# Attention and two mixture layers on one core: the experts' scores from operands split into a rounded and a low part

## The chip, the cores and the metric

The kernel runs on one core of one Trainium2 chip. The metric is the device time of one execution in microseconds (us), the median over several executions. Names of the engines: TensorE (PE, with its weight loads as PEld), VectorE (DVE), ScalarE (ACT), GpSimd (POOL), SyncE (SP).

## The reference

Three layers follow each other over a batch of 4, 576 positions and 512 features: a windowed attention of 8 heads, a gated feed-forward layer (products with `w_r`, `w_k`, `w_v`), and a layer of four attention experts with heads of 64. The last one is where the change is made:

```python
logits = x @ w_gate
topk = np.argpartition(-logits, K, axis=-1)[..., :K]      # K = 2
...
for e in range(E):                                        # E = 4
    q = x @ wq[e]
    k = x @ wk[e]
    v = x @ wv[e]
    scores = scale * (q @ k.transpose(0, 2, 1))
    scores = np.where(causal, -1000000000.0, scores)
    scores = scores - scores.max(-1, keepdims=True)
    a = np.exp(scores)
    a /= a.sum(-1, keepdims=True) + 1e-09
    ye = a @ v @ wo[e]
    ...
        out += mask[..., None] * w[:, :, kk:kk + 1] * ye
```

`wq` and `wk` are drawn large, so the scores are large numbers whose differences count.

## The kernel before, in words

Each engine has one program written out by hand, and semaphores order them. The batch loop runs four times. In one batch the dense stage (`pe_dense`) makes the gated layer for two halves of 288 positions, with the next batch's windowed attention put between its units; then comes the experts' stage (`pe_experts`).

All dense products and projections are made in three passes. `pe_passes` (L505 to L509) multiplies rounded by rounded (L507), rounded weights by low part (L508) and low weights by rounded (L509); both parts have the type float32r, and a low part is what rounding took away. The scores of the experts are made otherwise: keys and queries are kept as whole fp32 in `c_kq` and multiplied by a plain fp32 matmul, for which the trace shows two TensorE records each.

The experts' stage, in the order of TensorE:

- Projections, in the order of `PROJECTIONS`: kq 0 to 3, v 0 to 4, kq 4 to 7, twelve passes each. "kq n" is half n % 2 of the positions, of keys (n // 2 even) or queries (odd), for the pair of experts n // 4. They go through two PSUM banks `MM`; a bank may be filled again when `mm_out` of it has counted up, and ACT's `act_projection` (L851 to L863) empties it and counts: L863 writes `c_kq`, L859 writes `c_v`.
- Scores come in ten tiles k = 0 to 9 (`TILES`), five for each pair: 128 queries against 512, 384, 256 or 128 keys (`i` = 3, 2, 1, 0), and a last one (i = 4, at k = 2 and 6) of 64 queries against 576 keys. `pe_scores` (L593 to L618) makes one tile: the pair's two experts h = 0, 1 lie in partitions 0 to 63 and 64 to 127, so each tile is two matmuls with 64 rows (L612), and for i = 4 each head also has its own 64 columns (L606). A matmul of the mask closes the tile (L616, L608). Tile 0 is made after v 4, tile 1 after kq 7.
- After tile k: DVE takes the maximum (`c_negmax`, L1135), ACT the exponential and the sum (`c_prob`, L824), DVE the sum's inverse (L1141, L1145), POOL multiplies by inverse and gate (L1304), TensorE transposes (L640), ACT copies back (L837), and TensorE multiplies by v (L661). TensorE's order is scores k + 2, transposes k + 1, product with v of k; two score areas, `SC` for even and `MM` for odd k, are written in turn.
- DVE's order (`dve_experts`) is the first part of the gates, the maxima of tile 0, the second part of the gates, the sums of tile 0, then tile by tile.

The output product (`pe_out`) also goes through `pe_passes`, with 512 columns. Lines around the change:

```python
    for h in range(2):
        nc.tensor.matmul(score_area(k, h)[:, 0:(i + 1) * TC],
                         c_kq[own(h), 2 * pair + 1, i * TC:(i + 1) * TC],
                         c_kq[own(h), 2 * pair, 0:(i + 1) * TC], start=True, stop=False)
```

Of the kernel before, what the change touches and what calls it, by code (L numbers as in the profile page):

```python
# [27 lines left out]
def build(nc, qk, v, mu, w_k, w_v, w_r, c_v_w, c_k_w, c_q_w, c_o_w, out):  # L28
    fp32, f32r, bf16 = mybir.dt.float32, mybir.dt.float32r, mybir.dt.bfloat16
    ALU, ACT, AX = mybir.AluOpType, mybir.ActivationFunctionType, mybir.AxisListType  # L30

    B, PAIRS = qk.shape[0:2]
    H, S, D = HEADS, SEQ, HEAD_DIM
# [4 lines left out]
    SCALE = float(D) ** -0.5  # L38
# [3 lines left out]
    HALF = S // 2  # L42
# [6 lines left out]
    TC = 128  # L49
    LAST = S - TC * (NT - 1)  # L50
    SIZE = [TC] * (NT - 1) + [LAST]
    assert 2 * LAST == TC
    EP = E // 2
# [43 lines left out]
    def mm_index(what, n):  # L97
        return C0 + PROJECTIONS.index((what, n))
# [52 lines left out]
    PER_PAIR, LAST_STEP = 8, 8 * PAIRS + 2  # L151
# [29 lines left out]
    with ctx:  # L181
# [3 lines left out]
        def sem(name):  # L185
            return ctx.enter_context(nc.semaphore(name))

        def hl(name, shape):
            return sb(name + "_hi", shape, f32r), sb(name + "_lo", shape, f32r)
# [42 lines left out]
        def at(name, shape, dt, first):  # L232

            return nc.alloc_sbuf_tensor_at(name, shape, dt, offset=AREA0 + 4 * first)

        K2 = FT * HALF
# [40 lines left out]

        c_kq = at("c_kq", [128, 2 * EP, S], fp32, 2 * K2)  # L280
        cv = at("c_v", [TC, NT, NV], fp32, 2 * K2 + 3 * XR)
        assert 2 * K2 + 4 * XR + RING * HALF <= 10112 and NT * NV <= XR + RING * HALF
        assert 4 * S <= K2 and 2 * EP * S <= 2 * XR and 4 * S == K2

        c_negmax = sb("c_negmax", [TC, UNITS], fp32)
        c_sum = sb("c_sum", [TC, UNITS], fp32)
# [14 lines left out]
        MM = ctx.enter_context(nc.psum_tensor("MM", [128, 2 * BANK], fp32))  # L301

        def bank(t, n):
            return t[:, n * BANK:(n + 1) * BANK]
# [3 lines left out]
        const_ready = sem("const_ready")  # L308
# [24 lines left out]
        mm_out = [sem(f"mm_out{n}") for n in range(2)]  # L333
# [4 lines left out]
        pool_passed = sem("pool_passed")  # L338
        gate_step = sem("gate_step")
        gate_exp = sem("gate_exp")  # L340
        c_scored = sem("c_scored")
        c_max = sem("c_max")
        c_exp = sem("c_exp")
# [161 lines left out]
        def pe_passes(dst, w2, x2, first, last):  # L505

            nc.tensor.matmul(dst, w2[0], x2[0], start=first, stop=False)  # L507
            nc.tensor.matmul(dst, w2[0], x2[1], start=False, stop=False)  # L508
            return nc.tensor.matmul(dst, w2[1], x2[0], start=False, stop=last)  # L509
# [59 lines left out]
        def own(h):  # L569

            return slice(D * h, D * (h + 1))

        def score_area(k, h):

            return bank((SC, MM)[k % 2], h)
# [8 lines left out]
        def prob_tile(u):  # L584

            k, h, _, i = expert_tile(u)
            return cp[k % 2 * 2 + h][:, 0:(i + 1) * TC if i < NT - 1 else S]

        def pe_scores(pe, b, k):
            pair, i = TILES[k]  # L590
            m = SIZE[i]
            if k == 0:

                for n in (2, 3):
                    idx = mm_index("kq", n)
                    pe.wait_ge(mm_out[idx % 2], b * (MMS // 2) + idx // 2 + 2)
            if k >= 2:

                pe.wait_ge(c_exp, b * UNITS + TILE_UNITS[k - 2].stop)
            if i == NT - 1:  # L600

                cut = i * TC
                both = (SC, MM)[k % 2]
                for lo, hi in ((0, cut), (cut, S)):
                    for h in range(2):
                        nc.tensor.matmul(both[own(h), lo:hi], c_kq[own(h), 2 * pair + 1, cut:S],  # L606
                                         c_kq[own(h), 2 * pair, lo:hi], start=True, stop=hi <= cut)
                last = nc.tensor.matmul(both[:, cut:S], ident2[:, :, :].rearrange("p w n -> p (w n)"),  # L608
                                        causal[0:m, 0:m], start=False, stop=True)
            else:  # L610
                for h in range(2):
                    nc.tensor.matmul(score_area(k, h)[:, 0:(i + 1) * TC],  # L612
                                     c_kq[own(h), 2 * pair + 1, i * TC:(i + 1) * TC],
                                     c_kq[own(h), 2 * pair, 0:(i + 1) * TC], start=True, stop=False)
                for h in range(2):
                    last = nc.tensor.matmul(score_area(k, h)[:, i * TC:(i + 1) * TC], identb[:, :],  # L616
                                            causal[:, :], start=False, stop=True)
            last.then_inc(c_scored, 1)  # L618
# [236 lines left out]
        def act_projection(act_, b, what, n):  # L855
            idx = mm_index(what, n)
            act_.wait_ge(mm_full, b * MMS + idx + 1)
            if what == "v":
                nc.scalar.activation(cv[:, n, :], bank(MM, idx % 2)[0:TC, 0:NV], ACT.Copy)\  # L859
                    .then_inc(mm_out[idx % 2], 1)  # L860
                return
            half = n % 2
            nc.scalar.activation(c_kq[:, n // 2, half * HALF:(half + 1) * HALF], bank(MM, idx % 2)[:, 0:HALF],  # L863
                                 ACT.Copy, scale=SCALE if n // 2 % 2 else 1.0).then_inc(mm_out[idx % 2], 1)

        def act_experts(act_, b):

# [198 lines left out]
        def dve_r(dve, b, u):  # L1066

            if u not in R_AT:
                return
            half, n = R_AT[u]  # L1070
            r, of = 2 * (half * KT + n), half * (B_UNITS // 2) + n

            dve.wait_ge(mm_out[of % 2], b * (MMS // 2) + of // 2 + 2)
            g = gate_r[:, n, :]
            nc.vector.tensor_scalar_add(g, g, 1.0).then_inc(r_step, 1)
            dve.wait_ge(r_step, b * 4 * KT + r + 1)
            nc.vector.reciprocal(g, g).then_inc(r_step, 1)  # L1077
# [36 lines left out]
        def dve_gates_end(dve, b, step, settled):  # L1114
# [13 lines left out]
            for h in range(2):  # L1128
                one_each = g_exp[0:LAST, NT - 1, :].rearrange("r (p h) -> r p h", h=2)[:, :, h]
                step(nc.vector.tensor_tensor(gates_last[h * LAST:(h + 1) * LAST, :], one_each,  # L1130
                                             g_sum[0:LAST, NT - 1:NT].broadcast_to([LAST, EP]), ALU.mult))

        def dve_c_max(dve, b, u):
            dve.wait_ge(c_scored, b * PAIR_TILES + expert_tile(u)[0] + 1)
            nc.vector.tensor_reduce(c_negmax[:, u:u + 1], scores_of(u), AX.X, ALU.max,  # L1135
                                    negate=True).then_inc(c_max, 1)
# [10 lines left out]
        def dve_c_stat(dve, b, u):  # L1147
            dve_c_sum(dve, b, u)
            dve_c_inv(dve, b, u)
# [13 lines left out]
        def dve_experts(dve, b, ahead):  # L1163
            done = [0]

            dve_gates(dve, b, done, 0)
            for u in TILE_UNITS[0]:
                dve_c_max(dve, b, u)
            dve_gates(dve, b, done, 1)
            assert done[0] == GATE_STEPS  # L1170
            for u in TILE_UNITS[0]:
                dve_c_stat(dve, b, u)
            for k in range(1, PAIR_TILES):
                for u in TILE_UNITS[k]:
                    dve_c_max(dve, b, u)
                for u in TILE_UNITS[k]:
                    dve_c_stat(dve, b, u)
                if k == Y_SPLIT + 2:
                    dve_y_lo(dve, b, 0)
            if ahead:  # L1180

                for j in pieces_behind(1, -2)[0:2]:
                    dve_mix(dve, b + 1, j)
            dve_y_lo(dve, b, EP - 1)
            if ahead:
                for j in pieces_behind(1, -2)[2:]:
                    dve_mix(dve, b + 1, j)

                for j in pieces_behind(1, -1):
                    dve_mix(dve, b + 1, j)  # L1190

        def dve_batch(dve, b, ahead):
            for i in range(LAST_STEP):
                dve_dense(dve, b, i)
                if ahead:
                    dve_attention(dve, b + 1, i, (SOFT,))
                dve_r(dve, b, i)
                if ahead:
                    dve_attention(dve, b + 1, i, (SCORE, APPLY))
                for j in pieces_behind(b, i):  # L1200
                    dve_mix(dve, b, j)
                for c in lo_behind(b, i):
                    if DVE_MAKES_LO[c]:
                        dve_chunk(dve, c)
            dve_experts(dve, b, ahead)
# [111 lines left out]
        def _(pool):  # L1317
# [46 lines left out]
            for n in range(3):  # L1364
                pool.sem_inc(out_done[n], 1)
            pool.wait_ge(const_step, done)
            nc.gpsimd.affine_select(out=causal[:, :], in_=causal[:, :], compare_op=ALU.is_ge, fill=NEG,
                                    base=0, pattern=[[-1, TC]], channel_multiplier=1).then_inc(const_ready, 1)
            for p, o in FIRST_POOL:
                if p == "mix":  # L1370
                    pool_mix_lo(pool, 0, o)
                elif p == "lo":
                    pool_chunk(pool, o)
                else:
                    pool_step(pool, 0, p, o)
# [61 lines left out]
```

## Time and profile before

| | |
|---|---|
| median of 3 runs | 588.32 us (588.18 to 590.5) |
| the profiled execution, its time | 588.47 us |
| its span, first to last instruction | 586.7 us |
| granted TensorE clock, mean | 0.997 of full |
| busy: PE, PEld | 550.1 us, 482.5 us |
| busy: DVE, ACT, POOL | 340.7 us, 261.8 us, 233.0 us |

The profile is one execution. Its span leaves out 1.8 us at the two ends. Busy time of an engine is time in which at least one of its instructions runs; a matmul's record is longer than the time after which the next one starts, since they are pipelined. In rows of the trace, "<-" before an engine's name tells what ended the idle time before an instruction. "x4" counts instructions put into one row.

### The profile page before, as it was taken

To read this page: it belongs to the slowest core of one execution; us is meant where nothing else is said; L and a number is where in the kernel's file an instruction comes from. 1 tells how busy PE (TensorE), PEld (TensorE's weight loads), DVE (VectorE), ACT (ScalarE), POOL (GpSimd) and SP (SyncE) were. 2 spreads that over 40 slices of the span, in tenths; PEclk is the share of its full clock that TensorE was granted. 3 is DMA by queue.
4 is the path that set the end of the run, shared out by engine and by line. 5 is a ranking of instruction groups with operands and counts; after the bars stand their busy time and mean duration, and the time that the engine had idled before them with its cause. 6 is when DMAs were issued, how large, how long until landed. Compare 5 with 4: busy or idle time off the path is not lost.

```text
span 586.7 us, 12200 instructions
## 1 busy us (share of the span) xinstructions
PE 550.1 (94%) x5008; PEld 482.5 (82%) x5008; DVE 340.7 (58%) x696; ACT 261.8 (45%) x656; POOL 233.0 (40%) x285
## 2 busy tenths in 40 slices
PE   6789899999899999999989999999998999999987
PEld 5678789998559899999656999999965899999754
DVE  3998959613476882930458685582236866630451
ACT  2757544223664533322464553332256462322564
POOL 5658565311354641431235464133034554230241
PEclk9989999999999999999999999999999999999999
DMA  8980111200003112101002120100000200000002
GB/s 294 362 300 29 66 31 44 73 31 1 3 0 123 32 42 73 38 37 31 2 1 63 61 73 1 31 1 1 1 2 2 82 2 1 1 0 2 2 1 82
DMA packets 8935, 29.62 MB, mean 50 GB/s; under 512 B 1200, under 2 KB 1200, under 8 KB 8880
## 3 DMA queue, kind: packets, MB, share of 16 engines
q1 hardware_dynamic: 6256, 24.12, 12.5%
q10 hardware_dynamic: 2624, 4.72, 2.5%
q8 instruction: 40, 0.66, 0.5%
q14 instruction: 15, 0.12, 0.1%
HBM read 24.12 MB, written 4.72 MB: 49 GB/s over the span
## 4 chain that ended last, share of the span: by engine, by line
PE 74%; DVE 11%; POOL 6%; issue 4%; ACT 3%; DMA 1%; POOLq 0%
PE MM L507 20%; PE MM L509 18%; PE MM L508 18%; PE SC L465 4%; POOL c_prob L1304 3%; PE OA L661 3%; PE MM L612 3%; PE OA L496 2%; ACT c_prob L824 2%; PE TR L481 2%; DVE c_negmax L1135 2%; PE TR L640 2%; POOL prob L1247 1%; DVE row_inv L1000 1%; DVE mix L1032 1%
## 5 line engine op out<-in xcount | busy, mean ns | idle before, releaser
L1276 POOL TENSOR_TENSOR k_lo<-ring,k_hi 128x288 fp32r<-128x288 f32 x64 | 54.3, 850 | 98.4 <-ACT k_hi L805 98.4
L1304 POOL TENSOR_SCALAR c_prob<-c_prob,c_inv,gates 128x512 f32<-128x512 f32 (+3 forms) x64 | 41.9, 663 | 127.8 <-DVE c_inv L1145 127.8
L507 PE MATMUL MM<-k_hi,wv_hi 128*128 128x288 f32 x256 | 76.1, 297 | 4.8 <-DVE ring L1063 2.6
L507 PE MATMUL MM<-act_hi,wk_hi 128*128 128x288 f32 x256 | 77.4, 302 | 0.0
L508 PE MATMUL MM<-k_lo,wv_hi 128*128 128x288 f32 x256 | 75.5, 295 | 0.0
L508 PE MATMUL MM<-act_lo,wk_hi 128*128 128x288 f32 x256 | 75.4, 294 | 0.0
L509 PE MATMUL MM<-k_hi,wv_lo 128*128 128x288 f32 x256 | 75.3, 294 | 0.0
L509 PE MATMUL MM<-act_hi,wk_lo 128*128 128x288 f32 x256 | 75.2, 294 | 0.0
L1077 DVE RECIPROCAL gate_r<-gate_r 128x288 f32<-128x288 f32 x32 | 62.5, 1953 | 1.1
L1057 DVE TENSOR_TENSOR ring<-ring 128x288 f32<-128x288 f32 x64 | 41.5, 656 | 25.6 <-ACT ring L818 25.3
L1032 DVE SCALAR_TENSOR_TENSOR mix<-xT,one_less,mix 128x288 f32<-128x288 f32 x64 | 50.9, 796 | 7.3 <-ACT mix L918 6.2
L507 PEld LDWEIGHTS MM<-k_hi,wv_hi 128*128 128x128 f32 x256 | 48.0, 187 | 5.7 <-DVE ring L1063 3.3
L507 PEld LDWEIGHTS MM<-act_hi,wk_hi 128*128 128x128 f32 x256 | 48.1, 188 | 1.1
L508 PEld LDWEIGHTS MM<-act_lo,wk_hi 128*128 128x128 f32 x256 | 48.2, 188 | 0.0
L509 PEld LDWEIGHTS MM<-k_hi,wv_lo 128*128 128x128 f32 x256 | 48.2, 188 | 0.0
L509 PEld LDWEIGHTS MM<-act_hi,wk_lo 128*128 128x128 f32 x256 | 48.2, 188 | 0.0
L508 PEld LDWEIGHTS MM<-k_lo,wv_hi 128*128 128x128 f32 x256 | 48.1, 188 | 0.0
L818 ACT ACTIVATE ring<-MM 128x288 f32<-128x288 f32 x64 | 26.1, 408 | 48.7 <-PE MM L509 48.7
L640 PE MATMUL TR<-identf,c_prob 128*128 128x128 f32 (+1 forms) x200 | 34.7, 284 | 12.5 <-POOL c_prob L1304 10.9
L507 PE MATMUL MM<-xr_hi,wr_hi 128*128 128x288 f32 x128 | 40.0, 312 | 2.6 <-POOL xr_lo L1264 1.7
L1063 DVE TENSOR_TENSOR ring<-MM,gate_r 128x288 f32<-128x288 f32 x32 | 14.4, 451 | 42.6 <-PE MM L509 42.6
L508 PE MATMUL MM<-xr_lo,wr_hi 128*128 128x288 f32 x128 | 38.5, 300 | 0.0
(173 smaller groups left out, 1361.6 us busy)
## 6 DMA issues: line engine op xcount, KB each, us to landing
qkT<-in_qk SPq DMA_DIRECT2D x16, 591.5 KB, 3.9
vn<-in_v SPq DMA_DIRECT2D x16, 432.0 KB, 3.8
out_x<-c_prob ACTq DMA_DIRECT2D x16, 224.0 KB, 2.4
raw_wk_lo<-in_w_k SPq DMA_DIRECT2D x4, 512.0 KB, 16.2
raw_wv_lo<-in_w_v SPq DMA_DIRECT2D x4, 512.0 KB, 18.5
raw_wr_lo<-in_w_r SPq DMA_DIRECT2D x2, 512.0 KB, 8.5
out_x<-c_prob ACTq DMA_DIRECT2D x4, 256.0 KB, 2.4
raw_cv_lo<-in_c_v SPq DMA_DIRECT2D x1, 520.0 KB, 18.3
```

The costliest lines, as they stand in the source:

```text
L465: last = nc.tensor.matmul(tiles[rows, t, :], qT[rows, t * QA:(t + 1) * QA], kT[rows, t * QA:t * QA + KA], start=False, stop=t in (IN_BANK ...
L507: nc.tensor.matmul(dst, w2[0], x2[0], start=first, stop=False)
L508: nc.tensor.matmul(dst, w2[0], x2[1], start=False, stop=False)
L509: return nc.tensor.matmul(dst, w2[1], x2[0], start=False, stop=last)
L612: nc.tensor.matmul(score_area(k, h)[:, 0:(i + 1) * TC], c_kq[own(h), 2 * pair + 1, i * TC:(i + 1) * TC], c_kq[own(h), 2 * pair, 0:(i + 1) ...
L640: last = nc.tensor.transpose(turned_area(u)[0:SIZE[j], j * TC:(j + 1) * TC], prob_tile(u)[:, j * TC:j * TC + SIZE[j]], identf[:, :])
L818: nc.scalar.activation(ring[:, ITEM[u] % RING, :], src, ACT.Relu)\
L1032: nc.vector.scalar_tensor_tensor(out=slot, in0=xT[:, t, half * HALF:(half + 1) * HALF], scalar=one_less[:, m, t:t + 1], in1=slot, op0=ALU. ...
L1057: nc.vector.tensor_tensor(slot, slot, slot, ALU.mult).then_inc(squared, 1)
L1077: nc.vector.reciprocal(g, g).then_inc(r_step, 1)
L1276: nc.gpsimd.tensor_tensor(lo, ring[:, ITEM[u] % RING, :], hi.bitcast(fp32), ALU.subtract)\
L1304: nc.gpsimd.tensor_scalar(prob_tile(u), prob_tile(u), c_inv[:, u:u + 1], gate, ALU.mult, ALU.mult).then_inc(c_prob, 1)
```

## The change

Keys and queries get a rounded part (`c_kq_hi`, in the place of `c_kq`) and a low part (`c_kq_lo`, in a part of the area that the rounded k of the gated layer used before). ACT writes the rounded part of a projection from PSUM; then DVE computes the low part from PSUM and the rounded part (`dve_kq_lo`), and DVE, no more ACT, gives the bank back. Scores are three matmuls a head: rounded by rounded, rounded queries by low keys, low queries by rounded keys. The last 64 queries of a pair lie in `q_last`, a 128 x 128 block matrix with one head's queries in each corner of the diagonal and zeros beside them, which POOL fills once at the start; a tile of i = 4 is then three passes of full height for each of its two column ranges. For kq 3 and kq 7 the bank is read in three pieces, 224 columns of 128 partitions and two of 64 x 64.

```diff
-        c_kq = at("c_kq", [128, 2 * EP, S], fp32, 2 * K2)
+        c_kq = at("c_kq_hi", [128, 2 * EP, S], f32r, 2 * K2)
+        c_kq_lo = at("c_kq_lo", [128, 2, EP, S], f32r, 0)
...
+        q_last = hl("q_last", [128, EP, TC])
...
+        def kq_parts(n):
+            pair, q_or_k, half = n // 4, n // 2 % 2, n % 2
+            src, first = bank(MM, mm_index("kq", n) % 2)[:, 0:HALF], half * HALF
+            whole = HALF - LAST if (q_or_k, half) == (1, 1) else HALF
+            cols = slice(first, first + whole)
+            parts = [(c_kq[:, n // 2, cols], c_kq_lo[:, q_or_k, pair, cols], src[:, 0:whole])]
+            if whole < HALF:
+                parts += [(*[a[own(h), pair, own(h)] for a in q_last], src[own(h), whole:HALF]) for h in range(2)]
+            return parts
+
+        def c_parts(pair, q_or_k, h, cols):
+            return c_kq[own(h), 2 * pair + q_or_k, cols], c_kq_lo[own(h), q_or_k, pair, cols]
+
+        def pe_score_passes(dst_of, pair, queries, keys, closed):
+            for n, (x, y) in enumerate(((0, 0), (0, 1), (1, 0))):
+                for h in range(2):
+                    nc.tensor.matmul(dst_of(h), c_parts(pair, 1, h, queries)[x], c_parts(pair, 0, h, keys)[y],
+                                     start=n == 0, stop=closed and n == 2)
...
                 for lo, hi in ((0, cut), (cut, S)):
-                    for h in range(2):
-                        nc.tensor.matmul(both[own(h), lo:hi], c_kq[own(h), 2 * pair + 1, cut:S],
-                                         c_kq[own(h), 2 * pair, lo:hi], start=True, stop=hi <= cut)
+                    pe_passes(both[:, lo:hi], [a[:, pair, :] for a in q_last],
+                              [c_kq[:, 2 * pair, lo:hi], c_kq_lo[:, 0, pair, lo:hi]], True, hi <= cut)
...
-                for h in range(2):
-                    nc.tensor.matmul(score_area(k, h)[:, 0:(i + 1) * TC],
-                                     c_kq[own(h), 2 * pair + 1, i * TC:(i + 1) * TC],
-                                     c_kq[own(h), 2 * pair, 0:(i + 1) * TC], start=True, stop=False)
+                pe_score_passes(lambda h: score_area(k, h)[:, 0:(i + 1) * TC], pair,
+                                slice(i * TC, (i + 1) * TC), slice(0, (i + 1) * TC), False)
...
-            nc.scalar.activation(c_kq[:, n // 2, half * HALF:(half + 1) * HALF], bank(MM, idx % 2)[:, 0:HALF],
-                                 ACT.Copy, scale=SCALE if n // 2 % 2 else 1.0).then_inc(mm_out[idx % 2], 1)
+            for dst, _, src in kq_parts(n):
+                last = nc.scalar.activation(dst, src, ACT.Copy, scale=scale)
+            last.then_inc(c_kq_hi_out, 1)
...
+        def dve_kq_lo(dve, b, n):
+            dve.wait_ge(c_kq_hi_out, b * 4 * EP + n + 1)
+            if n % 4 == 3:
+                dve.wait_ge(q_last_zeroed, 2)
+            for hi, lo, src in kq_parts(n):
+                last = nc.vector.scalar_tensor_tensor(out=lo, in0=src, scalar=SCALE if n // 2 % 2 else 1.0,
+                                                      in1=hi.bitcast(fp32), op0=ALU.mult, op1=ALU.subtract)
+            last.then_inc(mm_out[mm_index("kq", n) % 2], 1)
...
+            for n in range(1, 4):
+                dve_kq_lo(dve, b, n)
             dve_gates(dve, b, done, 0)
             for u in TILE_UNITS[0]:
                 dve_c_max(dve, b, u)
+            dve_kq_lo(dve, b, 4)
             dve_gates(dve, b, done, 1)
+            dve_kq_lo(dve, b, 5)
             for u in TILE_UNITS[0]:
                 dve_c_stat(dve, b, u)
+            for n in range(6, 4 * EP):
+                dve_kq_lo(dve, b, n)
...
                 dve_r(dve, b, i)
+                if i == LAST_STEP - 1:
+                    dve_kq_lo(dve, b, 0)
...
+            pool.wait_ge(const_ready, 2)
+            for t in q_last:
+                nc.gpsimd.memset(t[:, :, :].bitcast(fp32), 0.0).then_inc(q_last_zeroed, 1)
```

The order of TensorE at the end of the projections, from the last pass of kq 7 to the mask of tile 2, in the first batch; first before (L612, L606 are scores, L640 transposes):

```order
L509 MATMUL MM<-act_hi,cq_lo 128x288
L507 MATMUL MM<-act_hi,cq_hi 128x288
L508 MATMUL MM<-act_lo,cq_hi 128x288
L509 MATMUL MM<-act_hi,cq_lo 128x288
L612 MATMUL MM<-c_kq 128x384 x2
L616 MATMUL MM<-causal,identb 128x128 x2
L640 MATMUL TR<-identf,c_prob_71 128x128 x4
L640 MATMUL TR<-identf,c_prob_72 128x128 x4
L606 MATMUL SC<-c_kq 64x512 x2
L606 MATMUL SC<-c_kq 64x64 x2
L608 MATMUL SC<-causal,ident 128x64
```

and with the change (L616 is now the score pass of one head, L643 the mask, L667 the transposes):

```order
L516 MATMUL MM<-act_hi,cq_lo 128x288
L616 MATMUL MM<-c_kq_hi 128x384 x2
L616 MATMUL MM<-c_kq_lo,c_kq_hi 128x384 x2
L616 MATMUL MM<-c_kq_hi,c_kq_lo 128x384 x2
L643 MATMUL MM<-causal,identb 128x128 x2
L667 MATMUL TR<-identf,c_prob_71 128x128 x4
L667 MATMUL TR<-identf,c_prob_72 128x128 x4
L514 MATMUL SC<-c_kq_hi,q_last_hi 128x512
L515 MATMUL SC<-c_kq_lo,q_last_hi 128x512
L516 MATMUL SC<-c_kq_hi,q_last_lo 128x512
L514 MATMUL SC<-c_kq_hi,q_last_hi 128x64
L515 MATMUL SC<-c_kq_lo,q_last_hi 128x64
```

The two fp32 matmuls of tile 1 have become six, and the two and two of tile 2 three and three over the whole array; nothing else of TensorE has moved.

The order of DVE from the maxima of tile 0 to those of tile 1; before:

```order
L1135 TENSOR_REDUCE c_negmax<-SC 128x1 x2
L1117 SCALAR_TENSOR_TENSOR g_exp<-g_dif,g_exp 128x20
L1120 TENSOR_REDUCE g_sum<-g_exp 128x5
L1122 TENSOR_SCALAR g_sum<-g_sum 128x5
L1124 RECIPROCAL g_sum<-g_sum 128x5
L1126 TENSOR_TENSOR gates<-g_exp,g_sum 128x20
L1130 TENSOR_TENSOR gates_last<-g_exp,g_sum 64x2 x2
L1141 TENSOR_SCALAR c_inv<-c_sum 128x1
L1145 RECIPROCAL c_inv<-c_inv 128x1
L1141 TENSOR_SCALAR c_inv<-c_sum 128x1
L1145 RECIPROCAL c_inv<-c_inv 128x1
L1135 TENSOR_REDUCE c_negmax<-MM 128x1 x2
```

and with the change, from the gates' last step on:

```order
L1160 TENSOR_TENSOR gates_last<-g_exp,g_sum 64x2 x2
L1169 SCALAR_TENSOR_TENSOR c_kq_lo<-MM,c_kq_hi 128x288
L1181 TENSOR_SCALAR c_inv<-c_sum 128x1
L1185 RECIPROCAL c_inv<-c_inv 128x1
L1181 TENSOR_SCALAR c_inv<-c_sum 128x1
L1185 RECIPROCAL c_inv<-c_inv 128x1
L1169 SCALAR_TENSOR_TENSOR c_kq_lo<-MM,c_kq_hi 128x288
L1169 SCALAR_TENSOR_TENSOR c_kq_lo<-MM,c_kq_hi 128x224
L1169 SCALAR_TENSOR_TENSOR q_last_lo<-MM,q_last_hi 64x64 x2
L1175 TENSOR_REDUCE c_negmax<-MM 128x1 x2
```

The low parts of kq 5, 6 and 7 stand between gates, sums and the next maxima; kq 7 has three instructions, on ACT too.

## Rows read from the trace of the kernel before

**Rows 1.** The page: busy time of TensorE; the chain that ended last, by engine, by line.
```profile
PE 550.1 (94%) x5008; PEld 482.5 (82%) x5008; DVE 340.7 (58%) x696; ACT 261.8 (45%) x656; POOL 233.0 (40%) x285
...
PE 74%; DVE 11%; POOL 6%; issue 4%; ACT 3%; DMA 1%; POOLq 0%
```

**Rows 2.** The chain in order of time: start, length, what; first batch, then fourth.
```profile
136.51 1.06 PE SC L612 x4
...
144.28 0.42 ACT c_kq L863
144.75 0.92 PE MM L612 x4
...
150.71 0.63 PE MM L612 x4
...
155.67 1.06 PE MM L612 x4
...
161.67 0.85 PE MM L612 x4
...
167.41 0.42 PE MM L612 x4
...
549.13 0.92 PE MM L612 x4
```

**Rows 3.** The timeline of TensorE: transposes of k = 0, tile 2, the next transposes.
```profile
145.72 1.04 PE L640 MATMUL TR<-identf,c_prob 128*128 128x128 f32 x8
146.69 1.19 PE L606 MATMUL SC<-c_kq 64*64 64x512 f32 x8
...
148.49 1.19 PE L640 MATMUL TR<-identf,c_prob 128*128 128x128 f32 x6 [0.48 <-POOL c_prob L1304]
```

**Rows 4.** The timeline of ACT: the emptying of kq 7.
```profile
144.28 0.41 ACT L863 ACTIVATE c_kq<-MM 128x288 f32<-128x288 f32 x1 [1.18 <-PE MM L509]
```

**Rows 5.** Line L612 in tile 0: durations in ns, least, median, most.
```profile
L612 PE MATMUL SC<-c_kq x4: 589/641/693, 136.4 to 137.0; 64*128 64x512 f32 x4
```

**Rows 6.** The chain in order of time: a pass of 288 columns, one of 512.
```profile
137.98 0.13 PE MM L508
...
172.38 0.23 PE MM L508
```

**Rows 7.** The timeline of ACT: two instructions in a row, the second on 64 partitions.
```profile
152.97 0.59 ACT L833 ACTIVATE c_probT<-TR 128x512 f32<-128x512 f32 x1
153.44 0.27 ACT L834 ACTIVATE c_probT<-TR 64x128 f32<-64x128 f32 x1
```

**Rows 8.** DVE, lines L1063, L1159 (ns, least/median/most), and L1106 in the timeline.
```profile
L1063 DVE TENSOR_TENSOR ring<-MM,gate_r x32: 395/456/458, 70.8 to 527.4; 128x288 f32<-128x288 f32 x32
...
L1159 DVE TENSOR_TENSOR k_hi<-OA,k_hi x4: 757/758/758, 172.7 to 576.6; 128x576 fp32r<-128x576 f32 x4
...
137.63 0.36 DVE L1106 TENSOR_TENSOR g_dif<-g_cmp 128x20 f32<-128x20 f32 x3
```

**Rows 9.** The timeline: ACT on kq 2 and 3, v 0's first pass, v 1's first.
```profile
127.80 0.41 ACT L863 ACTIVATE c_kq<-MM 128x288 f32<-128x288 f32 x1 [1.21 <-PE MM L509]
...
129.18 0.28 PE L507 MATMUL MM<-cv_hi,act_hi 128*128 128x260 f32 x1
...
129.38 0.41 ACT L863 ACTIVATE c_kq<-MM 128x288 f32<-128x288 f32 x1 [1.18 <-PE MM L509]
...
130.62 0.28 PE L507 MATMUL MM<-cv_hi,act_hi 128*128 128x260 f32 x1
```

**Rows 10.** The timeline: DVE's maxima of tile 0, gates' end; kq 7's first pass; POOL at the start.
```profile
138.43 1.28 DVE L1135 TENSOR_REDUCE c_negmax<-SC 128x1 f32<-128x512 f32 x2
...
140.57 0.33 DVE L1130 TENSOR_TENSOR gates_last<-g_exp,g_sum 64x2 f32<-64x2 f32 x2
...
142.50 0.30 PE L507 MATMUL MM<-act_hi,cq_hi 128*128 128x288 f32 x1
...
9.24 2.35 POOL L1313 TENSOR_TENSOR wr_lo<-raw_wr_lo,wr_hi 128x1024 fp32r<-128x1024 f32 x1 [1.72 <-ACT wr_hi L954]
```

**Rows 11.** Stretches: length, busy PE, PEld, DVE, ACT, POOL, granted clock, DMA share, GB/s.
```profile
30.30:34.60 4.30, 1.73 (x13) 1.48 (x12) 4.16 (x8) 3.22 (x5) 1.22 (x3) 1.00 1.03 418
34.60:38.30 3.70, 3.70 (x18) 3.51 (x17) 3.52 (x8) 0.59 (x2) 2.22 (x3) 0.54 1.03 318
142.70:146.10 3.40, 2.90 (x22) 2.12 (x21) 0.18 (x1) 0.82 (x2) 0.77 (x1) 1.00 0.00 0
```

More of the change, by code:

```diff
@@ L340, in build @@
         gate_exp = sem("gate_exp")
+        c_kq_hi_out = sem("c_kq_hi_out")
+        q_last_zeroed = sem("q_last_zeroed")
         c_scored = sem("c_scored")
@@ L861, in act_projection @@
                 return
-            half = n % 2
-            nc.scalar.activation(c_kq[:, n // 2, half * HALF:(half + 1) * HALF], bank(MM, idx % 2)[:, 0:HALF],
-                                 ACT.Copy, scale=SCALE if n // 2 % 2 else 1.0).then_inc(mm_out[idx % 2], 1)
+            scale = SCALE if n // 2 % 2 else 1.0
+            if n % 4 == 3:
+                act_.wait_ge(q_last_zeroed, 2)
+            for dst, _, src in kq_parts(n):
+                last = nc.scalar.activation(dst, src, ACT.Copy, scale=scale)
+            last.then_inc(c_kq_hi_out, 1)
         def act_experts(act_, b):
@@ L1131, in dve_gates_end @@
                                              g_sum[0:LAST, NT - 1:NT].broadcast_to([LAST, EP]), ALU.mult))
+        def dve_kq_lo(dve, b, n):
+            dve.wait_ge(c_kq_hi_out, b * 4 * EP + n + 1)
+            if n % 4 == 3:
+                dve.wait_ge(q_last_zeroed, 2)
[3 more added lines that the diff above has]
+            last.then_inc(mm_out[mm_index("kq", n) % 2], 1)
         def dve_c_max(dve, b, u):
```

## The prediction

> **What bounds the kernel now.** I began with the page. TensorE is busy 94% of the span, and the chain that ended last is 74% TensorE, but POOL's `c_prob`, DVE's `c_negmax` and ACT's `c_prob` are on it too [rows 1]. So the passes L507 to L509 are bound by TensorE, and the experts' softmax is bound by something longer than TensorE. The chain in order of time shows what. In a batch the chain holds the scores of tiles k = 0, 1, 3, 5, 7, 9 (1.06, 0.92, 0.63, 1.06, 0.85, 0.42 us), and between them maximum, exponential, sums, POOL's product and transposes; it leaves out k = 2, 4, 6, 8. The last batch repeats it to the hundredth [rows 2]. The even tiles end before POOL has made what the next transposes need: after k = 2, which took from 146.69, TensorE stands 0.48 us for `c_prob` [rows 3]. So what an even tile saves only lengthens such a wait, and six of ten tiles pay.
>
> At 144.28 ACT empties the last projection (kq 7) from PSUM, and TensorE waits for it before tile k = 1 [rows 2, 4]. That is the one place where the emptying of a projection is in sight, and the change makes that emptying longer.
>
> **The score passes.** From 128 to 512 key columns a tile grows from 0.42 to 1.06 us, in equal steps of 0.213 us for each 128 columns: four column times at 2.4 GHz, and 0.21 us left over that doesn't grow (1.06 less 4 x 0.213) [rows 2]. The four records of a 512-column tile are 589 or 693 ns long and all begin inside 0.6 us, so the two heads run side by side in the two halves of the array; the second pair has no waiting in it (589), the first one 104 ns [rows 5]. The left-over is therefore paid once a tile and stays.
>
> With rounded and low parts each head makes three passes of one column time instead of four. A pass of that kind costs 0.23 us for 512 columns and 0.13 for 288 [rows 6], by the line through both 0.175 for 384, 0.12 for 256, 0.065 for 128. If the two heads still run side by side, a tile is three of these and 0.21: 0.90, 0.74, 0.57, 0.41. The gain is 0.16 (k = 0 and 5), 0.18 (k = 1), 0.11 (k = 7), 0.06 (k = 3) and 0.01 (k = 9). At k = 9 it can be a loss of 0.18: eight transposes with 128 columns to load and 128 to stream take 1.04 us, 0.13 each, so three pairs may be bound by loading [rows 3]. The sum is 0.16 + 0.16 + 0.18 + 0.11 + 0.06 + 0.01 = 0.68, less half of that loss: I take **0.6 us a batch, 2.4 in all**. Upper end: a whole column time for each, 0.213 x (4 + 4 + 3 + 3 + 2 + 1)/4 = 0.91 a batch. Lower end: 0.68 - 0.18 = 0.5.
>
> The last 64 queries (k = 2 and 6) go from eight records in 1.12 us to six passes over the full array, about 3 x 0.23 + 3 x 0.06 + 0.1 = 1.0. Nothing waits for them: I count zero, and if the chain were TensorE alone it would be 0.1 each.
>
> **The emptying of kq 7.** Before, ACT's one instruction of 0.41 us [rows 4]. Now ACT makes three (224 columns, then two of 64 x 64), and then DVE three more. ACT: 128 x 512 takes 0.59, 128 x 288 0.41, so 224 columns 0.36 and 64 about 0.21; the next instruction starts 0.12 before the one before it ends (152.97 + 0.59 against 153.44) [rows 4, 7]. Together 0.24 + 0.09 + 0.21 = 0.54, **+0.13**. Lower end 0, as if it were one; upper end the plain sum 0.78, +0.37. DVE: reading PSUM and SBUF takes 456 ns at 288 columns and 758 at 576, so 0.39 at 224 and 0.22 at 64; back to back the three small ones of L1106 take 0.12 each though one is 0.17, 0.08 less for each that follows another [rows 8]. So 0.31 + 0.14 + 0.22 = 0.67, and one hand-over of 0.04 (ACT's end to TensorE at 144.75): **+0.71**. Lower end 0.50, as one instruction; upper end 0.87. The two together: **0.84 us a batch, 3.4 in all** (0.50 to 1.24). Nothing covers it: behind the waiting tile k = 1 stand on TensorE the transposes of k = 0 and tile k = 2, ready long before.
>
> **The emptying of kq 3.** It goes through the same bank as v 1, whose first pass starts at 130.62; ACT starts on kq 3 at 129.38 [rows 9]. 129.38 + 0.54 + 0.04 + 0.67 = 130.63, then TensorE's restart, 0.1 for a load that was ahead before: **0.11 us a batch, 0.4 in all** (0 to 0.5, with the upper ends above).
>
> **The rest at nothing.** kq 0, 1 and 2 are out of PSUM 0.3 to 0.6 us before their bank is wanted (kq 2: ACT from 127.80, DVE done at 128.7, v 0 at 129.18). DVE's two copies of x now come behind the low part of kq 0, 1.2 us later, and their only readers are late. kq 4 to 6: DVE ends the maxima of k = 0 at 139.71 and then does low part, 1.3 us of gates, low part: kq 5 is out at 142.2, and its bank is wanted at 142.5 [rows 10]; the cover is 0.3 us, and 0.16 of it goes when tile 0 gets faster. POOL's two fills of `q_last` fall into 1.72 us in which it waits for its first weights [rows 10]. The new tile in the area overlies the rounded k, which the projections no longer read.
>
> **Sum** against the profiled execution (588.47 us, beside a median of 588.32): -2.4 + 3.4 + 0.4 = +1.4, **589.9 us**. With all bounds it is from -0.91 x 4 + 0.50 x 4 = -1.6 to -0.5 x 4 + 1.74 x 4 = +5.0.
>
> **Rivals.**
> 1. *Each pass waits for its own weights* (slower). A load into a half of the array could be held until that half has finished its stream; then 0.104 us, the wait of the first pair [rows 5], stands before the second and third pass of every tile: 2 x 0.104 x 6 = 1.25 a batch, +5.0, 594.9. It decides once more than 0.16 per tile is added. Against it: the second pair of before has no such wait, and passes over the full array follow each other in 0.13. For it: those are other formats or shapes. The Trainium skill has this rule (TensorE: Matmul & The Clock Gate, "The mechanism" of Part 3: weights load under a running matmul only when the row group differs); by it the time is this 594.9; rows 5 and 6 speak against it. 12%.
> 2. *Rounded operands don't run side by side in the two halves.* No row shows that form on 64 partitions. Six passes in a row: 1.59 for 512 columns instead of 0.90, on the six tiles 3 x (0.23 x 2 + 0.175 x 2 + 0.12 + 0.065) = 3.0 a batch more, +12, 601.9. 8%.
> 3. *The clock falls.* TensorE's pause before k = 1 grows from some 0.5 to 1.4 us. The trace has one fall: after 4.3 us with 1.73 busy, the next 3.7 us ran at 0.54, the 1.2 GHz level. The stretch around k = 1 has 2.90 busy in 3.40 [rows 11]; with 0.9 more idle, two thirds. A spell like that one does 2.0 us of work in 3.7: 1.7 x 4 = 6.8, 596.7. 6%.
> 4. *Both emptyings at their upper ends*, a small operation on 64 partitions costing as much as its own plain duration: 593.5. 4%.
> 5. *The chain follows TensorE alone* (faster): all ten tiles pay one column time (3712 columns a batch, 1.55 us, 6.2 in all) and the kq 7 cost is at its lower end with no stall at v 1, 2.0: 584.3. Against it are the waits for `c_prob`. 10%.
> 6. That the change doesn't do what it says: the three kinds of passes stand in the order of instructions, so only a hidden wait could undo them; it is inside 1 to 4.
>
> **The numbers.** The sum has the other 60%: 589.9, and its bounds 586.9 to 593.5. A measurement of this kernel can tell about 0.5%, 2.9 us, from no change. Under 585.4 lies most of rival 5 and a little else: 11%. Over 591.3 lie rivals 1 to 4 with 30% and the upper part of the sum's own bounds, from which I take nothing more since half of that part is already rival 4: slower 31%, same 58%. For 8 in 10 the range runs from 586.5 to 596: it leaves out rival 2, rival 3 and rival 5's full price.
>
> **What would show it.** In the new profile a 512-column tile should stand with some 0.9 us, a 384-column one 0.74; TensorE's wait before k = 1 should be about 1.4 us in each batch and name DVE's `q_last_lo`; v 1 should begin 0.2 us late; the waits for `c_prob` behind k = 2 and k = 6 should grow by what those tiles save. The forecast is wrong if a 512-column tile takes over 1.1 (rivals 1, 2), if the granted clock in the experts' stage is below 1.00 (rival 3), or if the wait before k = 1 is under 0.8.

## The result, and the profile after

Five executions of the kernel before and five of the changed one ran beside each other.

| | before | after |
|---|---|---|
| median | 588.32 us (587.87 to 590.5) | 592.13 us (591.92 to 595.2) |
| ratio | | 1.0065, 95% interval 1.0048 to 1.0082 |
| span of the profiled execution | 586.7 us | 590.3 us |
| granted clock, mean | 0.997 | 0.997 |

The change costs 3.8 us, 0.65%. That lies inside the range of 586.5 to 596.0. It is 2.2 us above the forecast of 589.9, and beyond the 0.5% up to which I had called it the same, so the case with most of the chance (58%) missed and "slower" (31%) came. The sign of the sum was right; two of its terms were too small.

The page of the changed kernel, busy times and the chain by engine, against [rows 1]:

```profile
PE 548.4 (93%) x5056; PEld 491.3 (83%) x5056; DVE 356.8 (60%) x744; ACT 263.9 (45%) x672; POOL 233.5 (40%) x287
...
PE 72%; DVE 13%; POOL 6%; issue 4%; ACT 4%; DMA 1%; POOLq 0%
```

TensorE works 1.7 us less and the kernel is 3.6 us longer. DVE has 16 us more, but only what stands on the chain counts: its share there went from 11% to 13%.

The chain in order of time in the first batch (start, length, what), against [rows 2]:

```profile
137.34 0.90 PE SC L616 x6
...
144.91 0.36 ACT c_kq_hi L893
145.26 0.10 ACT q_last_hi L893
...
145.38 0.23 ACT q_last_hi L893
...
145.63 0.39 DVE c_kq_lo L1169
146.02 0.12 DVE q_last_lo L1169
...
146.16 0.24 DVE q_last_lo L1169
...
146.44 0.80 PE MM L616 x6
...
152.27 0.55 PE MM L616 x6
...
157.16 0.89 PE MM L616 x6
...
163.00 0.72 PE MM L616 x6
...
168.62 0.48 PE MM L616 x6
```

Between the last projection and the scores of tile k = 1 there was one link, of ACT; now there are six, of ACT and DVE. The score tiles are 0.90, 0.80, 0.55, 0.89, 0.72, 0.48 where they were 1.06, 0.92, 0.63, 1.06, 0.85, 0.42: gains of 0.16, 0.12, 0.08, 0.17, 0.13 and a loss of 0.06, together 0.60 a batch.

From ACT's start on kq 7 to TensorE's start on tile 1 it was 144.28 to 144.75, 0.47; now it is 144.91 to 146.44, 1.53. That is 1.06 a batch more. The timelines of ACT, DVE and TensorE there, against [rows 4]:

```profile
145.16 0.44 ACT L893 ACTIVATE q_last_hi<-MM 64x64 fp32r<-64x64 f32 x2
...
145.63 0.39 DVE L1169 SCALAR_TENSOR_TENSOR c_kq_lo<-MM,c_kq_hi 128x224 fp32r<-128x224 f32 x1 [1.41 <-ACT q_last_hi L893]
145.94 0.45 DVE L1169 SCALAR_TENSOR_TENSOR q_last_lo<-MM,q_last_hi 64x64 fp32r<-64x64 f32 x2
...
146.44 0.45 PE L616 MATMUL MM<-c_kq_hi 64*128 64x384 f32 x2 [1.57 <-DVE q_last_lo L1169]
```

TensorE's waits: releaser, microseconds in total, times, longest:

```profile
PE TR L667 <- POOL c_prob L1352: 11.0, 27, 0.9
PE MM L616 <- DVE q_last_lo L1169: 6.3, 4, 1.6
```

The second wait, in the kernel before:

```profile
PE MM L612 <- ACT c_kq L863: 2.0, 4, 0.5
```

It has grown by 4.3 us in four batches. The waits for `c_prob` were 10.9, 27 times, and have not moved.

The other place is v 1, which takes over the bank of kq 3, against [rows 9]: ACT, DVE and TensorE.

```profile
129.79 0.36 ACT L893 ACTIVATE c_kq_hi<-MM 128x224 fp32r<-128x224 f32 x1 [1.18 <-PE MM L516]
130.05 0.43 ACT L893 ACTIVATE q_last_hi<-MM 64x64 fp32r<-64x64 f32 x2
...
130.82 0.45 DVE L1169 SCALAR_TENSOR_TENSOR q_last_lo<-MM,q_last_hi 64x64 fp32r<-64x64 f32 x2
...
130.91 0.28 PE L516 MATMUL MM<-cv_hi,act_lo 128*128 128x260 f32 x1
131.33 0.39 PE L514 MATMUL MM<-cv_hi,act_hi 128*128 128x260 f32 x1
```

This execution's experts' stage began 0.41 us later than before's (ACT's kq 3 at 129.79 against 129.38), as its start varies from one execution to another (ACT's first `c_kq` at 124.20 before, 124.61 here, and at 124.20 in the second profile of the changed kernel, below). v 1's first pass began at 131.33 against 130.62, 0.30 later after that is taken off, and it is 0.39 long instead of 0.28, as after a pause: 0.41 a batch.

**The account.** -0.60 + 1.06 + 0.41 = +0.87 a batch, 3.5 us in four. The trace gives the same from outside: from ACT's first `c_kq` to the first output product of the batch it was 124.20 to 171.96, 47.76 us; it is now 124.61 to 173.22, 48.61 us, 0.85 more. The two profiled spans differ by 3.67 us: 3.26 of them lie behind ACT's first `c_kq`, and 0.41 before it, where the start varies as said.

### The profile page after: what moved, and what is told of

The parts are those of the page before. It is cut to its first block, busy times and chain, and to the rows that moved or that the text cites. A ratio compares the mean times of both kernels' runs of the same rounds, so it can differ in the third digit from the quotient of the medians.

```text
span 590.3 us, 12378 instructions
## 1 busy us (share of the span) xinstructions
PE 548.4 (93%) x5056; PEld 491.3 (83%) x5056; DVE 356.8 (60%) x744; ACT 263.9 (45%) x672; POOL 233.5 (40%) x287
## 4 chain that ended last, share of the span: by engine, by line
PE 72%; DVE 13%; POOL 6%; issue 4%; ACT 4%; DMA 1%; POOLq 0%
PE MM L514 19%; PE MM L516 17%; PE MM L515 17%; PE SC L472 4%; POOL c_prob L1352 3%; PE OA L688 3%; PE OA L503 2%; PE MM L616 2%; ACT c_prob L851 2%; PE TR L488 2%; DVE c_negmax L1175 2%; PE TR L667 2%; DVE row_inv L1030 1%; POOL prob L1295 1%; DVE mix L1062 1%
## 5 line engine op out<-in xcount | busy, mean ns | idle before, releaser
L667 PE MATMUL TR<-identf,c_prob 128*128 128x128 f32 (+1 forms) x200 | 34.9, 285 | 12.6 <-POOL c_prob L1352 11.0
L667 PEld LDWEIGHTS TR<-identf,c_prob 128*128 128x128 f32 (+1 forms) x200 | 20.9, 139 | 21.4 <-POOL c_prob L1352 21.1
```

What stands on the lines that cost most here:

```text
L667: last = nc.tensor.transpose(turned_area(u)[0:SIZE[j], j * TC:(j + 1) * TC], prob_tile(u)[:, j * TC:j * TC + SIZE[j]], identf[:, :])
```

## The experiments

My theory was that the passes give back 2.4 to 2.7 us and that the emptying of kq 7 and kq 3 costs more than that, by the time of small instructions. The rivals were a wait inside the tiles that makes the passes cheaper or dearer than a column time each, and an effect somewhere else in the batch. Below, "the kernel before" is the one that ran beside each experiment: 588.98 us in the first four, 588.99 in the last three. Times are medians with the least and the most.

### The passes alone

In the changed kernel:

```diff
-            whole = HALF - LAST if (q_or_k, half) == (1, 1) else HALF
+            whole = HALF
-            return c_kq[own(h), 2 * pair + q_or_k, cols], c_kq_lo[own(h), q_or_k, pair, cols]
+            return c_kq[own(h), 2 * pair + q_or_k, cols], c_kq[own(h), 2 * pair + q_or_k, cols]
-            last.then_inc(c_kq_hi_out, 1)
+            last.then_inc(mm_out[idx % 2], 1)
...
-            for n in range(1, 4):
-                dve_kq_lo(dve, b, n)
...
-            for n in range(6, 4 * EP):
-                dve_kq_lo(dve, b, n)
...
```

> The score passes alone. No low parts are computed: ACT empties each projection in one instruction and gives the bank back itself, as before the change, and the three passes all read the rounded part; the last 64 queries are left out (their block stays zero). Theory (the passes gain 0.6 us in each batch on the odd tiles and tile 0, the emptying costs more than that): faster than before by 4 x 0.6 = 2.4 us, 585.9, with a 512-column tile at 0.90 us and the waits for c_prob behind k = 2 and k = 6 longer. Rival (the passes gain nothing, because every tile's gain comes back as a wait, and the emptying is all that counts): 588.3.

Measured: 585.87 us (585.59 to 586.72), ratio 0.9946, interval 0.9931 to 0.996: 3.1 us faster. The chain from the emptying of kq 7:

```profile
143.85 0.42 ACT c_kq_hi L893
...
144.31 0.79 PE MM L616 x4
...
150.14 0.55 PE MM L616 x5
...
155.03 0.90 PE MM L616 x5
```

(Some records of a tile are missing from this trace, so it counts four or five of the six passes.) ACT to TensorE is 0.46 again, and the tiles have the lengths that they have in the changed kernel. From ACT's first `c_kq` to the end of the span it is 2.7 us less than before. The passes are a gain of their own, as the term said; that every tile's gain comes back as a wait is out.

### The emptying alone

Scores by plain fp32 as before, but ACT writes kq 3 and kq 7 in three pieces and DVE computes all low parts, which nothing reads:

```diff
-                parts += [(*[a[own(h), pair, own(h)] for a in q_last], src[own(h), whole:HALF]) for h in range(2)]
+                parts += [(c_kq[own(h), n // 2, S - LAST:S], q_last[1][own(h), pair, own(h)], src[own(h), whole:HALF])
+                          for h in range(2)]
...
-                pe_score_passes(lambda h: score_area(k, h)[:, 0:(i + 1) * TC], pair,
-                                slice(i * TC, (i + 1) * TC), slice(0, (i + 1) * TC), False)
+                for h in range(2):
+                    nc.tensor.matmul(score_area(k, h)[:, 0:(i + 1) * TC],
+                                     c_kq[own(h), 2 * pair + 1, i * TC:(i + 1) * TC],
+                                     c_kq[own(h), 2 * pair, 0:(i + 1) * TC], start=True, stop=False)
```

> The emptying alone. ACT and DVE treat the projections as in the change (kq 3 and kq 7 in three pieces each, DVE gives the bank back), but the keys and queries stay whole fp32 and the scores are the two fp32 matmuls of before; the low parts are written and not read. Theory: TensorE's wait before k = 1 grows by 1.06 us and v 1 begins 0.41 us late in each batch, 4 x 1.47 = 5.9 us, 594.2, and what this adds and what the passes alone save add up to the change's +3.8. Rival (the two parts aren't independent, and some of the loss comes from the passes themselves, as memory traffic or a lower clock): 590 to 592.

Measured: 595.15 us (594.86 to 596.21), ratio 1.0106, interval 1.0085 to 1.0127: 6.2 us slower. TensorE's wait before tile 1:

```profile
PE MM L643 <- DVE q_last_lo L1173: 6.3, 4, 1.6
```

The wait is the changed kernel's to the tenth, with fp32 scores behind it. The two halves add up: from ACT's first `c_kq` to the end of the span, the passes alone are 2.7 us shorter than before and the emptying alone 5.8 us longer, together +3.1; the changed kernel is 3.3 longer. So to within 0.2 us neither part acts through the other, and nothing else in that stretch has a price.

### One piece

The bank is emptied whole by one instruction of ACT and one of DVE; POOL copies the last 64 queries into the block matrix afterwards, from SBUF:

```diff
-            whole = HALF - LAST if (q_or_k, half) == (1, 1) else HALF
+            whole = HALF
+        def pool_q_last(pool, b, pair):
+            ...
+            for h in range(2):
+                for x in range(2):
+                    nc.gpsimd.tensor_copy(q_last[x][own(h), pair, own(h)],
+                                          c_parts(pair, 1, h, slice(S - LAST, S))[x]).then_inc(q_last_in, 1)
```

> The change with kq 3 and kq 7 emptied in one piece by ACT and one by DVE; POOL copies the last 64 queries, rounded and low, from the key and query tiles into the block, four copies of 64 x 64 for each pair, at times when it has nothing else to do. Theory (the three pieces cost 0.69 against 0.41 us on ACT and 0.77 against 0.46 on DVE, and all of it is in sight): 0.59 us less before k = 1 and no stall at v 1, 4 x 1.0 = 4.0 us off the change's 592.1, so 588.1, equal to before within 1 us. Rival (the wait is DVE's place in the order, not the length of its work): over 591.

Measured: 588.39 us (587.41 to 590.75), ratio 0.9989, interval 0.9975 to 1.0002: no difference from before, and 3.7 us under the changed kernel's 592.13 (by the two ratios to the kernel before, 4.5). ACT, DVE and TensorE at kq 7, and POOL's copies:

```profile
145.11 0.41 ACT L893 ACTIVATE c_kq_hi<-MM 128x288 fp32r<-128x288 f32 x1 [1.18 <-PE MM L517]
...
145.56 0.46 DVE L1167 SCALAR_TENSOR_TENSOR c_kq_lo<-MM,c_kq_hi 128x288 fp32r<-128x288 f32 x1 [1.13 <-ACT c_kq_hi L893]
...
146.07 0.44 PE L617 MATMUL MM<-c_kq_hi 64*128 64x384 f32 x2 [0.99 <-DVE c_kq_lo L1167]
...
146.08 0.23 POOL L1330 CAST q_last_hi<-c_kq_hi 64x64 fp32r<-64x64 f32 x1 [1.08 <-DVE c_kq_lo L1167]
...
146.96 0.23 POOL L1330 CAST q_last_lo<-c_kq_lo 64x64 fp32r<-64x64 f32 x1
```

From ACT to TensorE it is 0.96 in place of 1.53, so the splitting into three pieces costs 0.57 of the 1.06 and the low part as such the other 0.49. POOL's copies are over at 147.19, before it has `c_prob` of tile 1 to do. The wait at v 1 is gone too. Per batch 0.57 and the 0.41 of v 1 are 0.98, 3.9 us in all; from ACT's first `c_kq` to the end of the span the two kernels differ by 4.0. The changed kernel loses by reading the bank in pieces. DVE's place in its order has no part in it: DVE had been idle for 1.13 us when it began. The other 0.49 of the low part and the gain of the passes nearly cancel.

### The same half of the partitions

Both pieces of 64 x 64 are read from and written to partitions 0 to 63:

```diff
-                parts += [(*[a[own(h), pair, own(h)] for a in q_last], src[own(h), whole:HALF]) for h in range(2)]
+                parts += [(*[a[own(0), pair, own(h)] for a in q_last], src[own(0), whole:HALF]) for h in range(2)]
```

> The change with both small pieces of kq 3 and kq 7 on partitions 0 to 63; the second head's last 64 queries are left out, which costs no time by itself. Theory (two instructions that follow each other on different halves of the partitions don't overlap, which makes the second one full length): the two ACT pieces take 0.31 instead of 0.43 us together, DVE's 0.36 instead of 0.45, so 0.2 us less at both places in each batch, 4 x 0.4 = 1.7 off 592.1, 590.4. Rival (instructions of this size don't overlap whatever partitions they use): 592.1, with 0.43 and 0.45 for the two as in the change.

Measured: 590.61 us (589.59 to 593.74), ratio 1.0025, interval 1.0011 to 1.004: 1.5 us under the changed kernel's median, 2.4 by the ratios. The small pieces of ACT, then of DVE:

```profile
148.42 0.32 ACT L893 ACTIVATE q_last_hi<-MM 64x64 fp32r<-64x64 f32 x2
...
149.07 0.34 DVE L1169 SCALAR_TENSOR_TENSOR q_last_lo<-MM,q_last_hi 64x64 fp32r<-64x64 f32 x2
```

Two instructions of the same size take 0.32 and 0.34 together where they took 0.44 and 0.45. What is changed is in which half of the partitions the second one works, and with it that both now read the same 64 x 64 of the bank. It is 0.12 and 0.11, 0.23 at kq 7 and again at kq 3, so 1.8 us in four batches. TensorE's waits for `q_last_lo` fell from 6.3 to 5.3 us. The profiled execution was the longest of the twelve (593.74), and its experts' stage began only at 128.10, after a spell at the 1.2 GHz level from 18.3 to 32.0; from ACT's first `c_kq` to the end of the span it took 1.9 us less than the changed kernel. The experiment doesn't separate the half that is read from the half that is written. The two of L1130 [rows 10] both read partitions 0 to 63 and write first one half and then the other, and they don't overlap either: 0.15 each, and 0.33 together.

### A cover for the emptying, with passes and without

If the emptying is the cost, other TensorE work in front of the tile should hide it. On top of the one-piece kernel, TensorE makes tile 1 between kq 6 and kq 7 and tile 2 after kq 7, and kq 6 and 7 use the two banks `TR`:

```diff
+            return bank(TR if what == "kq" and n >= 6 else MM, mm_index(what, n) % 2)
...
+                if (what, n) == ("kq", 6):
+                    ...
+                    pe_scores(pe, b, 1)
+            pe_scores(pe, b, 2)
-            pe_scores(pe, b, 1)
...
-                if k + 2 < PAIR_TILES:
+                if 0 < k and k + 2 < PAIR_TILES:
```

ACT's exponentials of tile 1 and DVE's low part of kq 7 move with it, and POOL's copies for the second pair come one tile later. The same edit was made on the kernel before, with its fp32 scores. First the one with passes:

> The one-piece form with kq 6 and kq 7 made in the two banks of TR, which nobody uses then; tile 1 is made between kq 6 and kq 7 and tile 2 behind kq 7, so that passes of kq 7 and tile 2 lie over the emptying of kq 7 and over tile 1's softmax. Theory (the emptying costs only because nothing stands behind it, and the chain from tile 1 to its transposes is in sight): TensorE from the end of kq 7 to the end of tile 0's product with v takes 4.1 us and 1.0 for the tile made earlier instead of 6.65 in the one-piece kernel, 1.5 a batch, 6 us off 588.4: 582.4. Rival (the later tiles' chain takes up what the start gains): 586 to 588.

Measured: 583.22 us (582.39 to 584.5), ratio 0.9904, interval 0.9889 to 0.9918: 5.8 us under the kernel before and 8.8 under the changed one, which ran beside it. Then the one with fp32:

> The kernel before the change with the same new order: kq 6 and kq 7 in TR's banks, tile 1 between them, tile 2 behind kq 7; keys and queries whole fp32 and two matmuls a tile as before. Theory: the order gains about as much here less the emptying that it covers (0.5 us instead of 1.0 before k = 1), about 1.2 a batch, 583.5; the three passes are then worth 2 to 3 us once their emptying is covered, and covered_split is ahead by 1 to 3 us. Rival (fp32 tiles fill the same time without loss, so both are equal within 0.5).

Measured: 587.54 us (586.53 to 591.56), ratio 0.9984, interval 0.9969 to 0.9999: 1.4 us under before, where I had expected 5.5. That was a miss, and so was the lead of the form with passes: I had put it at 1 to 3 us, and it is 4.3. The chain from tile 1 to tile 3, of the fp32 form:

```profile
142.73 0.85 PE MM L615 x4
...
145.43 1.12 PE SC L609 x8
...
146.68 0.60 PE TR L643 x4
147.31 0.60 ACT c_probT L849
148.05 1.01 PE TR L643 x6
149.06 1.02 PE OA L664 x16
150.08 0.63 PE MM L615 x4
```

and of the form with passes:

```profile
142.19 0.72 PE MM L620 x6
...
144.77 0.23 PE SC L515
...
145.72 0.13 PE SC L642
145.85 0.66 PE TR L672 x4
...
146.54 0.60 ACT c_probT L878
...
147.28 1.01 PE TR L672 x6
148.28 1.02 PE OA L693 x16
149.31 0.55 PE MM L620 x6
```

In both, POOL's product and the emptying of kq 7 are off this stretch. What stands there instead is nearly all TensorE, with ACT's copy `c_probT` for the next transposes. Tile 1 used to have its softmax beside tile 2 and the transposes of tile 0; taking the softmax out leaves those to be done one after the other. In the fp32 form tile 3 starts at 150.08 where it started at 150.71 (with the stage 0.07 later): 0.70 a batch, 2.8 us. Not all of it reaches the measured time: from one batch's tile 0 to the next it is 0.46, 0.24 and 0.35 less than before (141.46, 141.83 and 120.04 against 141.92, 142.07 and 120.39), so 1.05 us of 2.1 is lost again between the stages. The trace shows where: at the end of the output product. ACT empties the output's banks into areas from which an earlier output transfer must have left, and waits for that transfer; the gated layer's first product waits for ACT's bank. In the second batch:

```profile
320.11 0.60 ACT L909 ACTIVATE c_prob<-MM 112x512 f32<-112x512 f32 x1 [1.86 <-DMA out_x<-c_prob]
...
320.75 0.40 PE L507 MATMUL MM<-xr_hi,wr_hi 128*128 128x288 f32 x1 [0.36 <-ACT c_prob L909]
```

In the first and third batch ACT waits 1.48 and 1.59 us at this row, for such a transfer too. In the profiled execution before, it waits 0.78 for TensorE at this row, and in the second batch for the transfer only one row later. Whether this belongs to the form or to the one execution that was profiled is not shown. The form with passes has no such loss (1.40, 1.57 and 1.41 less, for 1.38 in the stage).

With passes the batch's stretch from ACT's first `c_kq` to the output product is 46.38 us against 47.06, so 0.68 shorter still: of tiles on the chain -0.17, -0.13, -0.17 (tile 2: 144.77 to 145.85, 1.08, against 145.43 to 146.68, 1.25), -0.08, -0.16, -0.13 and +0.06, which makes 0.78, and 0.1 lost between them. Tile 2 pays here, since in this order the transposes follow it at once and TensorE has no wait between them. That is 2.7 of the 4.3 us between the two kernels, and the loss of 1.05 that only the one profile has would be most of the rest.

### The change again

> The change itself once more, beside the others on one chip. It should stand 3 to 4 us above before, and its stretch from ACT's first kq to the end 3.2 us above that of before, as in the first profile.

Measured, beside the last two: 592.01 us (591.26 to 593.97), ratio 1.0059, interval 1.0042 to 1.0076. ACT's first `c_kq` is at 124.20, the first output product at 172.82: 48.62 us, as in the first profile of the change (48.61).

## Why the prediction was partly right and partly wrong

**The score passes: right.** I took 0.6 a batch; it is 0.60. The tiles of 0.90, 0.74, 0.57, 0.41 came as 0.90, 0.72, 0.55, 0.48. Tile 1 is 0.80: I had set the 0.92 of before, which has 0.07 of restart after a pause in it (tile k = 7 of the same size had 0.85), against a tile without that. At k = 9 the loss is 0.06, inside the bound of 0.18 that I gave it.

**The emptying of kq 7: the mechanism right, the size 0.84 instead of 1.06 a batch.** Here is the step that failed. I took each piece as overlapping the one before it: by 0.12 on ACT, as the pair of [rows 7], and by 0.08 on DVE, as the three small ones of L1106 [rows 8]. DVE's low parts became 0.76 instead of 0.67, ACT's rounded ones 0.69 instead of 0.54. The first 64 x 64 piece does overlap the 224 columns before it, on ACT by 0.10. The second begins only when the first has ended: on ACT the first is on from 145.16 to 145.36, and the second from 145.38 to 145.60. The better row stood beside the ones that I used: the two of L1130, which write first one half of the partitions and then the other, take 0.33 together [rows 10], with no overlap. The three of L1106 are on all 128 partitions, and the second of the ACT pair works on half of those of the first; the row to take was the one in which the halves alternate as here. The same-half experiment shows that it is this: 0.44 to 0.32, 0.45 to 0.34. Over two engines that is 0.23, and the step missed 0.22. The mechanism stood; the term that was mis-sized is the length of the second 64 x 64 piece.

**The emptying of kq 3: 0.11 instead of 0.41 a batch.** The same step again. ACT's pieces took 0.15 more than I had set and DVE's 0.09; the last 0.06 are from DVE's end (131.27) to TensorE's start (131.33), which I had left out here. Together 0.30. I had put DVE's end within 0.01 us of the point at which the cover is used up, so the whole of that error came through as a wait.

**The sum.** The two are 0.22 + 0.30 = 0.52 a batch, 2.1 us, and 589.9 + 2.1 = 592.0; measured were 592.13 and 592.01.

**What I counted at nothing was nothing.** POOL's two fills of `q_last` stand at 7.58 and 7.83, 0.31 each, and its first `wr_lo` begins at 9.19 as before (9.24), after waiting 1.05 us. kq 5's low part is done at 142.70; its bank is wanted at 143.12, when kq 7's first pass begins. The passes alone and the emptying alone add up to the whole within 0.2 us, which leaves little room for more.

**One sign did not show.** I said that the waits behind k = 2 and 6 would grow by what those tiles save. From tile 2's start to the idle time it is 1.33 us (148.09 to 149.42) against 1.32 before: it saves nothing there. Its first pass is 0.47 long instead of the 0.40 of the others. The wait behind k = 2 grew from 0.48 to 0.64 since tile 2 began 1.65 us after tile 1 instead of 1.94, while `c_prob` came only 0.12 sooner. The total for `c_prob` stayed, since in the same batch later waits for it shrank by 0.02 to 0.06 each (0.30 to 0.24, 0.89 to 0.86, 0.21 to 0.18, 0.25 to 0.23). Nothing hung on it.

**The rivals.** *Each pass waits for its own weights* fell. Line L616 in tile 0 (durations in ns, least/median/most, and starts):

```profile
L616 PE MATMUL SC<-c_kq_hi x2: 493/494/494, 137.3 to 137.3; 64*128 64x512 f32 x2
L616 PEld LDWEIGHTS SC<-c_kq_lo,c_kq_hi x2: 186/186/186, 137.4 to 137.4; 64*128 64x128 f32 x2
L616 PE MATMUL SC<-c_kq_lo,c_kq_hi x2: 392/392/393, 137.6 to 137.6; 64*128 64x512 f32 x2
...
L616 PE MATMUL SC<-c_kq_hi,c_kq_lo x2: 393/393/393, 137.8 to 137.8; 64*128 64x512 f32 x2
```

The second pair's weights load from 137.4 on, while the first pair (137.3 and 0.49 long) is on. Only the first pair has the 0.10 of waiting. By the rule of the Trainium skill (TensorE: Matmul & The Clock Gate, "The mechanism" of Part 3) the load of a pass would wait for the stream before it in the same half; with the 0.104 of rows 5 for each of two waits, an estimate, a 512-column tile would be 1.11. It is 0.90, so here the measurement decides against it. At 128 columns the tile became 0.06 longer, not shorter: its passes begin 0.16 and 0.11 apart, over the 0.06 that I had set, and each has a load of 0.19. That the loads hold them is likely, but no run shows it. *No running side by side* fell with the same rows: six passes in a row would be 1.59. *The clock falls* fell too. A stretch of the changed kernel, in the columns of [rows 11]:

```profile
143.00:148.50 5.50, 3.93 (x33) 3.40 (x32) 2.39 (x8) 1.51 (x5) 1.52 (x2) 1.00 0.01 1
```

With 1.57 us of idle time in it the clock is at 1.00, the 2.4 GHz level. *Both emptyings at their upper ends* was the nearest to what happened: 1.06 and 0.41 of its 1.24 and 0.5. Its cause, small operations at their own plain duration, is right for the second piece and not for the first. I had 4% on it. *The chain follows TensorE alone* fell: TensorE's busy time went down and the time went up. *That the change doesn't do what it says* fell by the passes alone.

The chances were off for one reason: 2.2 us of error in the sum is 0.4%, and the sum stood 1.4 us from the bound of "slower" at 591.3. I had said "from which I take nothing more" of the upper part of the sum's own bounds, though they reached to 593.5. Bounds of 0.50 to 1.24 and 0 to 0.5 around 0.84 and 0.11 lie more to the upper side, at kq 3 above all, and that part should have had a chance of its own.

## What to carry to other kernels

Before a buffer is emptied by two engines in turn, look for the one place where the reader waits for it directly: an added step is free where something covers it and costs its full time four times over where nothing does. Keep such an emptying to one instruction an engine and let an idle engine rearrange the result from SBUF; here that was worth about 4 us, and putting other TensorE work in front of the reader about 5 more. When work is moved to cover a wait, add up what then stands on the chain instead: with fp32 scores 1.4 us came where I had expected 5.5.

## What the runs showed of the hardware

- Two instructions in a row on ACT or on DVE overlapped when they worked on the same 64 partitions (two of 64 x 64 in 0.32 and 0.34 us) and did not when the second worked on the other 64 (0.44 and 0.45 us). One on 64 partitions did begin before one on all 128 had ended, by 0.10 us on ACT (145.16 against 145.26) and by 0.08 on DVE (145.94 against 146.02).
- A product of 64 rows in three passes of float32r operands ran side by side in both halves of the array as fp32 did: 0.90 us for 512 columns and two heads against 1.06. At 128 columns it was the slower one, 0.48 against 0.42.
- In a 512-column tile the weights of the second pass loaded under the first pass's stream in the same half of the array (from 137.4, the stream on from 137.3 for 0.49 us), and the passes followed each other by 0.23 to 0.34 us (137.26, 137.60, 137.83).
